# A convolution and two feed-forward layers on one core: products of the first tile moved to the lower half of TensorE, and the unread products at the end taken out

## The reference

```python
w = exp(weight_gen - max); w = w / (sum(w) + 1e-09)        # over the 7 taps
x1 = einsum('bshk,bskhg->bshg', w, windows of 7 tokens of x)   # 8192 tokens x 192
h = maximum(x1 @ w_in, 0.0);  x2 = h * h @ w_out               # layer 1
h = x2 @ w_in2;               out = (h * cos(h)) @ w_out2      # layer 2
```

## Time and profile before

| what | us |
|---|---|
| median of 3 runs | 1177.59 (1177.59 to 1177.81) |
| profiled execution | 1177.56 |
| span of its profile | 1175.7 |
| TensorE busy | 1172.7 |
| DVE busy | 960.4 |
| ACT busy | 806.1 |
| GpSimd busy | 366.3 |

### The profile page before, as it was taken

One profiled execution on the slowest core, in us unless ns is written; L12 is line 12 of the kernel. 1 busy time (PEld: TensorE's weight loads), 2 busy tenths in 40 slices (PEclk: granted clock), 3 DMA queues, 4 the chain that ended last, 5 costly groups with the idle time before them and its releaser, 6 DMA issues.

```text
span 1175.7 us, 25787 instructions
## 1 busy us (share of the span) xinstructions
PE 1172.7 (100%) x9953; PEld 1132.5 (96%) x9954; DVE 960.4 (82%) x1504; ACT 806.1 (69%) x1467; POOL 366.3 (31%) x265
## 2 busy tenths in 40 slices
PE   9999999999999999999999999999999999999999
PEld 7989999999999999999999999999999999999988
DVE  7968899878878787887878878787787878878787
ACT  4977666667667666666766666676666767666676
POOL 4993634070420706125070430705215070000000
DMA  8511111110111101111011111101111000100001
GB/s 214 135 51 30 35 28 35 17 37 15 23 35 28 35 11 19 35 28 35 15 19 34 25 35 28 35 9 21 35 28 35 13 17 3 26 2 15 1 1 28
DMA packets 113174, 37.33 MB, mean 32 GB/s; under 512 B 101662, under 2 KB 110878, under 8 KB 113052
## 3 DMA queue, kind: packets, MB, share of 16 engines
q1 hardware_dynamic: 111100, 34.87, 14.2%
q10 hardware_dynamic: 1952, 0.80, 0.3%
HBM read 23.84 MB, written 6.29 MB: 26 GB/s over the span
## 4 chain that ended last, share of the span: by engine, by line
PE 100%; issue 0%; DVE 0%
PE y L608 51%; PE h L608 46%; PE y L713 1%; PE h L630 1%; PE h L1121 0%; PE h L637 0%; PE y L674 0%; PE h L640 0%; PE h L644 0%; PE h L1123 0%; PE y L675 0%; PE y L676 0%; PE y L725 0%; DVE g_hi L1543 0%; PE y L659 0%
## 5 line engine op out<-in xcount | busy, mean ns | idle before, releaser
L608 PE MATMUL y<-g_hi,wo 64*128 64x512 f32 x3048 | 698.2, 393 | 0.2
L608 PE MATMUL y<-g_lo,wo 64*128 64x512 f32 x2032 | 521.1, 391 | 0.0
L608 PEld LDWEIGHTS y<-g_hi,wo 64*128 64x128 f32 x3048 | 420.5, 184 | 14.5 <-PE y L608 1.1
L529 POOL TENSOR_TENSOR tap<-xc,gen 128x768 f32<-128x768 f32 x98 | 150.9, 1546 | 575.3 <-DVE xd_lo L1522 555.2
L608 PEld LDWEIGHTS y<-g_lo,wo 64*128 64x128 f32 x2032 | 305.3, 184 | 2.0
L1179 ACT ACTIVATE turns<-turns 128x512 f32<-128x512 f32 x238 | 150.2, 631 | 182.4 <-DVE turns L1473 182.4
L608 PE MATMUL h<-xa_hi,wa_hi 64*128 64x512 f32 x1018 | 270.6, 397 | 0.1
L608 PE MATMUL h<-xa_hi,wa_lo 64*128 64x512 f32 x1018 | 266.0, 391 | 0.0
L608 PE MATMUL h<-xa_lo,wa_hi 64*128 64x512 f32 x1018 | 265.5, 391 | 0.0
L1493 DVE TENSOR_TENSOR h<-h,turns 128x512 f32<-128x512 f32 x238 | 165.6, 696 | 114.6 <-ACT turns L1179 114.2
L1467 DVE SCALAR_TENSOR_TENSOR h<-h,relu 128x512 f32<-128x512 f32 x249 | 173.4, 696 | 57.2 <-ACT relu L1154 55.0
(11 more groups left out here) (127 smaller groups left out, 1092.7 us busy)
## 6 DMA issues: line engine op xcount, KB each, us to landing
xc<-in_x_dram SPq DMA_DIRECT2D x60, 240.0 KB
out_dram<-arena SPq DMA_DIRECT2D x62, 64.0 KB, 1.9
xt_a<-x_blocks SPq DMA_DIRECT2D x224, 16.0 KB, 1.8
arena<-in_moe_w_out_dram SPq DMA_DIRECT2D x16, 192.0 KB, 3.7
arena<-in_moe_w_in_dram SPq DMA_DIRECT2D x16, 128.0 KB, 2.5
out_dram<-arena SPq DMA_DIRECT2D x62, 32.0 KB, 1.7
xt_d<-x_blocks SPq DMA_DIRECT2D x112, 16.0 KB, 1.8
arena<-in_moe_w_in_dram SPq DMA_DIRECT2D x16, 64.0 KB, 2.9
```

The source lines that it names most:

```text
L529: pool.tensor_tensor(tap[:, k % 2, :].rearrange("p (r g) -> p r g", g=GROUP), rows[k], wk, ALU.mult).then_inc(pool_step, 1)
L608: return pe.matmul(o, w[rows, :], x[rows, :], start=start, stop=stop)
```

## The change

Three things are edited.

1. In slots 3 to 15 of tile 0, one `up_d` product (even slots) or two (odd slots) are no longer issued on TOP but on BOTTOM, by a new function `up_d_bottom` at the end of the slot. To make that possible, transfers copy rows 0 to 63 of `wd_lo`, of the odd blocks of `wd_hi` and of tile 0's `xd_hi` to rows 64 to 127: 64, 32 and 128 KB each. SyncE issues them between its loads, two for each weight piece 1 to 7 and one for the tokens.
2. The first `up_a` BOTTOM of the slot, with its wait on `h1_left`, stands ahead of the first `down_a` TOP instead of behind it.
3. The 16 unread products at the end are gone.

```diff
+        def moved_down(n):
+            return () if not HEAD_D1 <= n < SLOTS else (0, 1) if n % 2 else (1,)
...
+            def copy_head_weights(pc):
+                cols, odd = slice(pc * PIECE, (pc + 1) * PIECE), slice(pc * PIECE + P, (pc + 1) * PIECE)
+                sp.wait_ge(piece_ready[pc], 2)
+                for w, at in ((wd_lo, cols), (wd_hi, odd)):
+                    sp.dma_start(w[DD:P, at].bitcast(F32), w[0:DD, at].bitcast(F32)).then_inc(head_w_copied[pc], 16)
...
             for pc in range(RING, RING + 2):
                 load_piece(pc)
+                copy_head_weights(pc - RING + 1)
+            sp.wait_ge(x1_hi_ready, 2)
+            sp.dma_start(xd_hi[DD:P, 0, :].bitcast(F32), xd_hi[0:DD, 0, :].bitcast(F32)).then_inc(head_x_copied, 16)
             load_gen(sp, 2)
             for pc in range(RING + 2, PL + 4):
                 load_piece(pc)
+                if pc - RING + 1 < PL:
+                    copy_head_weights(pc - RING + 1)
...
+            def up_d_bottom(o, f, k, **group):
+                w = wd_lo if k == 1 else wd_hi
+                return half(o, w[:, f * P:(f + 1) * P], xd_hi[:, 0, :], BOTTOM, **group)
...
+                moved = moved_down(n)
+                kept = [k for k in range(3) if k not in moved]
...
                     last = down_a(down, BOTTOM, k, start=k == 0)
-                    last_up = up_d(o, 0, i, par, k)
+                    if k < len(kept):
+                        last_up = up_d(o, 0, i, par, kept[k])
...
+                pe.wait_ge(h1_left, n - HEAD_D1 + 1)
+                up_a(o, 0, i, par, BOTTOM, 0)
                 pe.wait_ge(y1_a_left, downs_in_halves(down_of_slot(n)))
                 down_a(down, TOP, 0)
-                pe.wait_ge(h1_left, n - HEAD_D1 + 1)
-                up_a(o, 0, i, par, BOTTOM, 0)
+                up_a(o, 0, i, par, BOTTOM, 1)
                 down_a(down, TOP, 1)
-                up_a(o, 0, i, par, BOTTOM, 1)
+                last_up = up_a(o, 0, i, par, BOTTOM, 2, stop=not moved)
+                if moved:
+                    pe.wait_ge(head_x_copied, 16)
+                    pe.wait_ge(head_w_copied[i // PF], 32)
+                for k in moved:
+                    last_up = up_d_bottom(o, i, k, stop=k == moved[-1])
+                last_up.then_inc(up1_done, 1)
                 down_a(down, TOP, 2, stop=True).then_inc(down1_done, 1)
-                up_a(o, 0, i, par, BOTTOM, 2, stop=True).then_inc(up1_done, 1)
...
-            spare = g2_hi[:, 0, :]
...
-            for j, moving in enumerate((line, pairs, lines)):
-                for _ in range(4):
-                    pe.matmul(h[:, j, :], wo[1][:, j, 0:P], moving, start=True, stop=True)
-            for _ in range(4):
-                pe.matmul(h[:, 3, :], wo[1][:, 3, 0:DD].bitcast(mybir.dt.bfloat16),
-                          spare[:, 0:TOK // 2].bitcast(mybir.dt.bfloat16), start=True, stop=True)
```

More of the change, by code:

```diff
@@ L241, in conv_ffn_ffn_kernel @@
         w_copied = sem("w_copied")
+        head_w_copied = [sem(f"head_w_copied{pc}") for pc in range(PL)]
+        head_x_copied = sem("head_x_copied")
         y1_summed = sem("y1_summed")
@@ L1114, in _ @@
                 tail_slot(n)
-            spare = g2_hi[:, 0, :]
-            line = spare[:, 0:4].unsqueeze(1).to_broadcast([P, TOK // 4, 4])
-            pairs = spare.rearrange("p (b n two) -> p n b two", b=2, two=2)
-            lines = spare.rearrange("p (b n four) -> p n b four", b=2, four=4)
-            for j, moving in enumerate((line, pairs, lines)):
-                for _ in range(4):
-                    pe.matmul(h[:, j, :], wo[1][:, j, 0:P], moving, start=True, stop=True)
-            for _ in range(4):
-                pe.matmul(h[:, 3, :], wo[1][:, 3, 0:DD].bitcast(mybir.dt.bfloat16),
-                          spare[:, 0:TOK // 2].bitcast(mybir.dt.bfloat16), start=True, stop=True)
         @block.scalar
```

## The result

The changed kernel takes 1179.96 us in the median of 22 runs (1177.84 to 1182.62), the kernel before 1177.59 (1177.43 to 1177.9, 22 runs): a ratio of 1.0019, with a 95% interval of 1.0012 to 1.0025. It is slower by 2.4 us, above the range of the prediction. The runs of the changed kernel also lie 4.8 us apart, those of the kernel before 0.5. The profiled execution took 1181.29 us, its span 1179.5.

A forecast was written before the change was run, and what follows sets the result against it. TensorE was taken as the bound (busy 1172.7 of 1175.7 us), with ACT and DVE nearly full in the head. 0.3 us lost up to the transposes, 0.70 saved behind them, end 0: 1177.56 - 0.4 = 1177.2, range 1175.0 to 1179.4.

The forecast's parts named there:

- The first transfer: Slot 3: the copy of xd_hi, issued at 22.8 to 23.2, lands at 27.8, so slot 4 starts 1.6 us later.
- The count of bytes: Token copy's landing: 1562 kB outstanding at 20.83, moved at 223 GB/s, take 7.0 us, a landing at 27.8.
- The fit that the prediction takes: One DMA as about 2.0 us plus bytes over 436 GB/s: 2.3 us for the token copy and no stall.
- The price of a late landing: Slots 3 to 13: each microsecond of landing behind 27.8 reaches the transposes whole; slower than before from 28.2 on.
- late rival: Slot 3: the token copy queues 7.6 us and lands at 30.4, net +2.2 us, 1179.8; chance 0.22.
- ACT and DVE: Slots 4 to 13: their chain puts the transposes at 52.3 instead of 52.01, +0.3 us, the saving there gone.
- the check on ACT: Relu 7 to 17: ACT's times put relu 17 at 64.6 and layer 2's input at 69.4, just covered by 69.5.
- The moved products: Slots 3 to 15: 20 steps of 0.233 us leave the upper half, at most 4.67 us off TensorE.
- the rival with unbalanced halves: Slots 3 to 15: the halves do not balance, each slot costs 10 steps; 1177.4, no change; chance 0.08.
- They cost nothing: SyncE's queue: copies of later pieces, issued 5 us or more before their slot, and the loads behind them cost 0.
- The end: Last 5 us: removing the unread products leaves the stores' path as it is, 0, bounds 0.1 either way.
- The in-time case: Slot 3: the token copy lands by 25.8, transposes come 1.66 us earlier, slots 14 and 15 save 0.70: 1175.2; chance 0.18.

The follow-up runs named there:

- e2: The changed kernel with the 16 unread products put back at the end: 1179.88 us.
- e4: The changed kernel with 14 unread products filling TensorE's gap in slot 3, ahead of the wait for the token copy: 1180.08 us.
- e16: The changed kernel with GpSimd's shift of part 4 one piece earlier and the first late weight piece loaded ahead of tile 2's rows (both reliefs): 1179.39 us.
- e6: The changed kernel with products moved only from slot 6 on, transfers as they are: 1178.38 us.
- e10: e9 with both reliefs (GpSimd's shift of part 4 one piece earlier, first late weight piece loaded ahead of tile 2's rows): 1175.96 us.
- e9: e6 without the weight copies of pieces 1 and 2, pieces 4 and 5 loaded back to back, then the token copy and piece 3's copies: 1176.79 us.
- e5: The changed kernel with all its transfers and its order of products, but no product moved: 1177.58 us.
- e1: The kernel before without the 16 unread products at the end, nothing else: 1177.50 us.
- e3: The changed kernel with the token copy issued from ACT right behind its source's rounding and the weight copies one load earlier each: 1179.24 us.
- e17: e10 with GpSimd's second kind of operation in tile 2's convolution held back until DVE has made xd_lo: 1175.94 us.
- e13: The changed kernel with only the token copy moved, issued from ACT right behind its source's rounding: 1178.44 us.

## Why the prediction was wrong

- **The first transfer: this step failed first.** The issue was put at 22.8 to 23.2; it is at 24.94, for the most part since piece 4 went out 0.56 later and the second `wd_lo` copy took 1.52 us to issue where I counted 0.5 to 0.6. The landing was put at 27.8; five profiles of kernels with this queue have 27.8 (e2), 28.4 (e4), 28.8 (e16), 29.1 (e6) and 29.35 (changed). The forecast is the lucky end of what happens, reached in e2 with an issue at 24.6. The count of bytes was fair (216 GB/s where I used 223); that an issue can take much longer was left out, though the earlier trace rows had one of 1.78 us at 22.82. The fit that the prediction takes from the Trainium skill, page "DMA: Bandwidth & Descriptors", section "Anatomy of one DMA — SWDGE (gpsimd) path", is given there for transfers on GpSimd's path. This copy goes out from SyncE, and it took 3.2 to 4.4 us in the five profiles.
- **The price of a late landing.** "Each microsecond behind 27.8 reaches the transposes whole" holds (e4's slot 4 starts 1.48 us behind e2's, its transposes at 53.90 are 1.46 behind e2's 52.44), and more comes on top: relu 4 was 2.92 us later than the forecast's 30.77, 1.5 of it the landing and 1.4 the clock, which no part of the forecast had. My late rival priced a landing at 30.4 at 2.2 us; in the profiled run 29.35 with the low clock cost 3.7, in e2's 27.8 without it 0.8.
- **ACT and DVE.** With the landing at 27.8 (e2) this chain was right to a tenth as far as relu 7 (forecast 38.88, measured 38.95) and the transposes (52.3, measured 52.44, right behind DVE's addition, which ends at 52.34). It failed behind them: relu 17 at 65.51 instead of 64.6, layer 2's first product at 70.68 instead of 69.5. The exp of part 4 waited 1.76 us for GpSimd. That is the second failed step. I wrote of three nearly full engines; the earlier trace rows has four, with 20.10 us of GpSimd. Two smaller slips: the check on ACT leaves out relu 11's wait of 0.26 us (47.25 in the kernel before), so its relu 17 would be at 64.3, and layer 2's input came 5.11 us after relu 17, not 4.77, with `xd_lo` at 1.60 us.
- **The moved products (up to 4.67 us off TensorE).** The term was mis-sized. These are the first upper products of slots 8, 9 and 10 in e10:

```profile
36.15 0.39 PE L630 MATMUL h<-xa_hi,wa_hi 64*128 64x512 f32 x1
...
38.57 0.39 PE L630 MATMUL h<-xa_hi,wa_hi 64*128 64x512 f32 x1
...
40.76 0.39 PE L630 MATMUL h<-xa_hi,wa_hi 64*128 64x512 f32 x1
```

An even slot costs 2.42 us and an odd one 2.19, and the changed kernel has the same (38.25, 40.44, 42.87). A pair costs 4.62 where two slots of 2.57 cost 5.13: 0.51 us back, not the 0.70 of three steps. By these rows slots 3 to 15 save an estimated 3.5 us, not 4.67, and slots 6 to 15 in e10 2.6, not 3.5, of which 2.0 reach the end in its profile and 1.5 in the median. The odd slot, under ten steps (2.33), shows that the halves do run ahead of each other; the pair is nevertheless at the 20 steps (4.66) of the rival with unbalanced halves. In each slot one product on each half starts 0.30 to 0.33 us behind the one before it instead of 0.23, and what holds it is not shown. The new place of the first lower product costs nothing by itself, as forecast: e10's slots 4 and 5, which have it and move nothing, take 2.57.

- **"They cost nothing" (the later copies and the loads behind them).** Wrong for one copy, by 1.08 us in e6's profile, and perhaps by the 1.4 us between the medians of e6 and e9, though true where nothing is moved (e5).
- **The end.** Right: e1.
- **The rivals.** The late case named the right direction, with 0.22, and its 1179.8 is close to the median by luck: it had a landing at 30.4 and no clock, the profiled run has 29.35 and the low clock. The in-time case (1175.2) is refuted as worked out: with the copies in time the kernel took 1179.24, and 1176.18 once two waits on other engines were gone.

In sum, the changed kernel pays a gap of 1.9 to 3.5 us in slot 3 (three profiles), in its long form 1.4 more for the clock, and gets back little, since from slot 12 on a GpSimd shift and a weight landing hold ACT. Four kernels put that in numbers, as distances from the kernel before: with the late copy +2.4 and +1.95 us (without and with reliefs), with copies in time +1.7 and -1.3. Taking either obstacle away alone yields 0.4 or 0.7 us in the median, which is hardly clear of the spread; both together yield 3.6, which is. What lengthens single runs by 1 to 3 us where there is no gap (e3, e6, e9, e17) stays open.

The best version is e10 or e17 (products moved from slot 6, no copies that nobody reads, the first late piece ahead of the rows): 1175.96 and 1175.94, 1.5 to 1.7 below the kernel before, each with a ratio to it of 0.9988 (0.9979 to 0.9997), and about 4 below the changed kernel.

## What to carry to other kernels

A chain that reads "TensorE 100%" names the engine that is last now; before you forecast a gain, list every engine whose row has next to no idle time in that stretch (four here) and every landing whose reader follows within a microsecond, because each can take over in turn. A transfer put into a backed-up queue can cost its issuer time as well (1.52 us once here), and its landing differed by 1.5 us between five profiles: give it a reader that comes well behind the worst one, and drop the copies that feed nobody. Here the spread of the runs grew tenfold with the change, and the gap behind a transfer was what made it: a grown spread is worth following up as much as the median. And measure what a moved product gives back: a count of steps promised 0.70 us a pair, the rows gave 0.51.

## What the hardware did that I had not expected

- TensorE's granted clock fell to 0.61 and 0.53 in the two windows behind a wait of 3.49 us and was back at 1.00 by 34; behind the waits of 1.93 us (e2) and 2.67 us (e16), and with the gap filled (e4), it stayed at 1.00.
- A DVE subtraction of two SBUF operands took 0.69 us alone and up to 2.32 beside a GpSimd operation, and ended 0.55 us after it. The Trainium skill, page "SBUF — State Buffer", section "SBUF: two separate sides", has it that a DVE operation with two SBUF inputs and a GpSimd operation that reads SBUF contend for a shared pair of ports under an exclusive lock, and that the later one stands still until the first is through. The e13 and e17 rows agree.
- A 64 KB copy inside SBUF took SyncE 1.52 us to issue at 22.73 in the changed kernel and 0.48 at 29.38. The DMA share was 1.15 from 22 to 24 us and 1.09 from 28 to 30, so busy DMA engines alone don't make an issue slow; what does is not shown.
